# Three of the six hole-filling transfers of a later group move from ScalarE's program to SyncE's

## The reference

```python
for t in range(S):                                   # B, H, S, D = 4, 8, 768, 48
    cur = einsum('bhd,bhe->bhde', u[None] * kt, vt)
    y[:, :, t] = einsum('bhd,bhde->bhe', rt, state + cur)
    state = wt[..., None] * state + einsum('bhd,bhe->bhde', kt, vt)
x = y.transpose(0, 2, 1, 3).reshape(B * S, H * D)    # 3072 x 384
h = x @ w_in                                         # 384 x 2048
x = maximum(0.01 * h, h) @ w_out                     # 2048 x 384
# then: softmax over 8 experts by cosine / tau, argmax, and
out[mask] = gate_w[mask, None] * (maximum(x[mask] @ w1[e], 0) @ w2[e])   # F = 1024
```

## Time and profile before

| what | value |
|---|---|
| median of 3 runs | 859.35 us (857.68 to 860.33) |
| the profiled execution | 861.14 us |
| its span | 859.3 us, 17826 instructions |
| mean granted clock of PE | 0.993 |
| busy PE / DVE / ACT / POOL | 824.3 / 547.6 / 438.5 / 198.8 us |
| PE, L967 (1152 matmuls) and L988 (1152) | the first network, up to 573 us |
| PE, L1040 and L1076 | the experts, from 573 us to the end |

### The profile page before, as it was taken

One profiled execution on the slowest core, in us unless ns is written; L12 is line 12 of the kernel. 1 busy time (PEld: TensorE's weight loads), 2 busy tenths in 40 slices (PEclk: granted clock), 3 DMA queues, 4 the chain that ended last, 5 costly groups with the idle time before them and its releaser, 6 DMA issues.

```text
span 859.3 us, 17826 instructions
## 1 busy us (share of the span) xinstructions
PE 824.3 (96%) x5689; PEld 773.5 (90%) x5689; DVE 547.6 (64%) x1296; ACT 438.5 (51%) x919; POOL 198.8 (23%) x285
## 2 busy tenths in 40 slices
PE   5789999999999999999999999999999999999995
PEld 5689999999999999999999989999889988988885
DVE  6687598678778778878868855645461422454462
ACT  4565464364465455446446436554563534465472
POOL 5421011003012112112112001212323332423443
PEclk9999999999999999999999999999999999999998
DMA  8795221238122122112220000513531513285381
GB/s 176 160 233 127 52 65 39 44 76 89 38 69 38 39 60 56 39 24 69 44 43 30 2 15 29 167 37 102 193 112 40 186 38 131 98 295 181 110 275 49
DMA packets 141576, 78.81 MB, mean 92 GB/s; under 512 B 111566, under 2 KB 129525, under 8 KB 141362
## 3 DMA queue, kind: packets, MB, share of 16 engines
q1 hardware_dynamic: 134786, 64.69, 29.7%
q0 software_dynamic: 4544, 10.85, 3.8%
q10 hardware_dynamic: 2160, 2.21, 1.4%
HBM read 112.90 MB, written 11.63 MB: 145 GB/s over the span
## 4 chain that ended last, share of the span: by engine, by line
PE 79%; DVE 5%; DMA 3%; ACTq 3%; issue 3%; ACT 1%; SPq 0%; POOLq 0%; POOL 0%; DVEq 0%
PE bank L988 20%; PE bank L967 19%; PE bank L1076 12%; PE bank L1040 12%; ACTq L423 3%; PE bank L896 3%; PE bank L924 3%; PE bank L864 2%; PE bank L1057 2%; DMA xg<-x_moe,gi 2%; PE bank L919 2%; PE bank L904 1%; PE bank L1022 1%; DVE Xi L1527 1%; DVE Fi L1516 1%
## 5 line engine op out<-in xcount | busy, mean ns | idle before, releaser
L967 PE MATMUL bank<-xhl,WRh 128*128 128x384 f32 x768 | 218.7, 339 | 2.7 <-DMA xhl<-xhl 2.7
L967 PEld LDWEIGHTS bank<-xhl,WRh 128*128 128x128 f32 x768 | 141.4, 188 | 3.5 <-issue 2.0
L1311 ACT COPY gw<-bank 128x384 f32<-128x384 f32 x128 | 61.5, 481 | 155.1 <-PE bank L967 154.4
L988 PE MATMUL bank<-WRh,gh 128*128 128x384 f32 x384 | 136.4, 355 | 0.0
L967 PE MATMUL bank<-xhl,WRl 128*128 128x384 f32 x384 | 130.1, 339 | 0.0
L988 PE MATMUL bank<-WRh,gl 128*128 128x384 f32 x384 | 129.7, 338 | 0.0
L988 PE MATMUL bank<-WRl,gh 128*128 128x384 f32 x384 | 129.6, 338 | 0.0
L1597 DVE TENSOR_TENSOR gl<-gw,gh 128x384 fp32r<-128x384 f32 x128 | 76.2, 595 | 55.4 <-ACT gh L1317 51.9
L1590 DVE SCALAR_TENSOR_TENSOR gw<-gw 128x384 f32<-128x384 f32 x128 | 71.2, 556 | 61.5 <-ACT gw L1311 61.5
L1317 ACT CAST gh<-gw 128x384 fp32r<-128x384 f32 x128 | 65.4, 511 | 85.3 <-DVE gw L1590 59.4
L1765 DVE TENSOR_TENSOR hl<-bank,hh 128x512 fp32r<-128x512 f32 x56 | 36.1, 686 | 85.3 <-ACT hh L1352 83.4
(11 more groups left out here) (191 smaller groups left out, 1597.3 us busy)
## 6 DMA issues: line engine op xcount, KB each, us to landing
stage<-in_moe_w_dram SPq DMA_DIRECT2D x96, 768.0 KB
Wn<-in_w_dram SPq DMA_DIRECT2D x24, 192.0 KB, 2.6
Rn<-in_r_dram SPq DMA_DIRECT2D x24, 192.0 KB, 3.4
Kn<-in_k_dram SPq DMA_DIRECT2D x24, 192.0 KB, 3.5
Vn<-in_v_dram SPq DMA_DIRECT2D x24, 192.0 KB, 2.6
x_moe<-x2s SPq DMA_DIRECT2D x24, 192.0 KB, 2.8
wraw<-in_moe_w_out_dram SPq DMA_DIRECT2D x4, 768.0 KB, 7.8
eraw<-in_moe_w_dram SPq DMA_DIRECT2D x4, 768.0 KB, 9.7
```

Of the source, the lines that this page charges most:

```text
L967: mm = pe.matmul(bank[F_BANK[n % 2]][:, 0:GN], win(t_)[:, f // 4, k_, cols], xhl[G % 2][:, a, k_, :], start=(k_ == 0 and n_ == 0), stop=(k ...
L988: mm = pe.matmul(bank[O_BANK[i]][:, 0:DM], a[:, z, cols], wout(t_)[:, f, :], start=(f == 0 and n_ == 0), stop=(f == FT - 1 and n_ == 2))
L1311: act.copy(gw[:, n % 2, :], bank[F_BANK[n % 2]][:, 0:GN]).then_inc(s_g0, 1)
```

## The change

`fill` of SP is new: it waits for `s_yhi` and `s_ylo` of group g and issues `fill_half(sp, g, 1)`. It is called for group 0 where the same lines stood, and for groups 1 to 7 at the point of SP's program at which the third chunk's sums are due, ahead of `next_v`. ACT's `fill` loses its second `fill_half`. The number of transfers, their sizes and what waits for them (`s_fill`) are as before.

```diff
+            def fill(g):
+
+                sp.wait_ge(s_yhi, GT * (g + 1))
+                sp.wait_ge(s_ylo, GT * (g + 1))
+                fill_half(sp, g, 1)
...
-            sp.wait_ge(s_yhi, GT)
-            sp.wait_ge(s_ylo, GT)
-            fill_half(sp, 0, 1)
+            fill(0)
...
             for n in range(SECOND):
                 for m in at(sum_at, n - 1):
+                    if m % GT == GT - 1:
+                        fill(m // GT)
                     if m + NSLOT < NC:
                         next_v(m + NSLOT)
...
                 fill_half(act, g, 0)
-                if g > 0:
-                    fill_half(act, g, 1)
```

## The result

| | before | after |
|---|---|---|
| median, 6 runs each | 858.64 us (857.68 to 860.33) | 853.78 us (852.95 to 855.45) |
| ratio | | 0.9942, 95% interval 0.993 to 0.9953 |
| profiled execution, its span | 861.14, 859.3 us | 855.45, 853.7 us |
| PE from the matmul at 60.11 (61.89 after) to the first of the experts, below "the first stage" | 513.04 us | 508.20 us |
| from there to the end of the span | 286.2 us | 283.6 us |

A forecast was written before the change was run, and what follows sets the result against it. PE, with work for 96% of the span, was taken as the bound, its gaps hanging on ACT's six issues in a row. The gains 2.94 + 0.15 + 1.55 = 4.64 us, from 859.35, gave 854.7 us, range 852.6 to 857.8.

The forecast's parts named there:

- (a): Six gaps before PE's scores, behind the fills of groups 1 to 6: all closed, 2.94 us gained.
- (b): Start of group 6: the last fill lands 1.9 us earlier, 0.15 us gained.
- (c): Start of group 7: PE reads the flag and branches under running matmuls, 1.55 us gained.
- (d): SP issues three more fills in seven places, its load of v goes out 3.2 us later: cost 0.
- (e): Landing of fills issued by SP and ACT at once: still in time for PE, cost 0, bounds 0 and 0.9.
- Another holder of `Kt`: Before the scores: the six gaps stay, only 1.70 us gained, 857.7 us; chance 0.10.
- Nothing to be seen: Experts' stage: PE comes 4.6 us earlier but loses it to transfers keeping their own time, 859.35 us; chance 0.09.
- Flag not covered: Start of group 7: PE's sequencer can't branch ahead of its matmuls, gain there 0.56, 855.7 us; chance 0.16.
- Slower: Groups 1 to 6: ACT's fills and the load of v slow each other; 863.6 us with landings of 6; chance 0.05.

The follow-up runs named there:

- the held kernel: The changed kernel plus eight small copies on ACT behind its three fills, holding ACT for 1.76 us with no transfer; ratio 0.9961 to before.
- the one with the scans first: The kernel before, with DVE doing the decay scans ahead of the low part that waits for ACT, all six fills left on ACT; ratio 0.9972.

## Why the prediction was right

The time, 853.78 us, lies 0.9 us under the forecast of 854.7 and in the range. The forecast was taken from a median of before of 859.35, which six runs put at 858.64; against its own reference the gain was 4.86 us where 4.64 were forecast.

**(a) The gaps before the scores** were all closed, 2.28 + 0.64 = 2.92 us for 2.94. The reading of the chain from ACT's issue over DVE's low part to `Kt` was right, as the held kernel and the one with the scans first show from two sides. What I gave as the limit in groups 3 to 6, the router's products on DVE, was there, but tighter than I had it. Group 5 after, and below it `Kt` of the same group before:

```profile
371.65 1.90 ACTq L423 DMA_DIRECT2D xhl<-xhl  x3
374.81 0.08 DVE L1616 DVE_READ_ACCUMULATOR2_ANT logits<- 128x1 f32 x1
374.81 1.35 DVE L1603 TENSOR_TENSOR gl<-gw,gh 128x384 fp32r<-128x384 f32 x1
381.40 0.68 DVE L1550 TENSOR_TENSOR Kt<-bank,Xi 128x512 f32<-128x512 f32 x1
```

```profile
371.72 3.83 ACTq L423 DMA_DIRECT2D xhl<-xhl  x6
381.98 0.68 DVE L1544 TENSOR_TENSOR Kt<-bank,Xi 128x512 f32<-128x512 f32 x1
```

The low part starts 1.3 us earlier, as I had said, but directly behind the products it takes 1.35 us and not 0.56. From ACT's first issue, `Kt` comes 9.75 us later where it was 10.26, so only 0.51 us of ACT's 1.92 arrive, and not 1.25. It is the same in groups 3 and 4; in group 6, whose last issue had been stretched, it is 0.93. The gap was 0.46. PE's scores now start 0.20 us behind the end of `Kt` where they had waited until 0.15 behind it: in groups 3 to 6 there is 0.05 us to spare, and not the 0.79 that 1.25 would leave. In group 1, without the products, it is 1.46. That the gaps of groups 3 to 6 closed in full is in part luck. It is also why one transfer moved does as much there as three: in that kernel `Kt` of groups 3 to 6 comes at 9.73 or 9.74 us.

**(b) Group 6's start** gave its 0.15. The gap was put down to the landing, rightly, but not explained: it was an issue of 1.02 us, met by chance of the code's layout. Part of the 0.64 in (a) has the same source. These 0.3 us belong to the change as it is, and would not be there in a kernel whose code lies otherwise.

**(c) The branch** gave 1.56 us for 1.55. This was the step with two outcomes, and the one that I took came in: PE's sequencer read the flag and branched under nine matmuls. Choosing the flag and not the transfer that the profile names was right, and mattered: with the flag out of the way and the transfers as they were, PE waits 0.77 us less, which is how far apart the two paths ended.

**(d), (e) SP and the landings** cost nothing. SP's load of v was issued 3.4 us later (103.36 less the 1.78 of the whole picture, against 98.20), with no wait behind it. The cost of running beside the fills, which I bounded at 0 to 0.9, is 0.5 us of landing time and none of PE's. In that bound I took the issue of 1.02 us for what two sequencers cost each other. That was wrong: ACT issued alone there, and the packet above came with it. In group 0, where SP and ACT issue together, the longest was 0.81 us before and 0.87 after.

**The rivals.** "Another holder of `Kt`" is out by the gaps. "Nothing to be seen" is out by the time: the experts' stage did not get longer (286.2 us, then 283.6), and the kernel is faster, clear of the interval. "Flag not covered" is out: 0.17 us and not 1.2. "Slower" needed landings of 5.3 us; 3.3 was the longest. The rule that the prediction quotes from the Trainium skill ("DMA: Bandwidth & Descriptors", section "Issuing engines are not separate DMA queues"), that starting transfers from several engines saves only the sequencer's time, was weighed and set aside; the trace agrees with the rule itself, as the transfers got no faster (2.2 us, and 2.7 beside a load). It is its closing remark, that this time is small, that did not carry over: the whole gain came from 1.9 us of a sequencer's time, seven times.

## What to carry to other kernels

Issuing a transfer costs the engine that issues it as much as a small instruction, here 0.64 us each, and six in a row stand in that engine's program ahead of all that follows. Count such rows of issues as work where the engine has a deadline, and follow what its next instruction feeds, through the other engines' program order, until PE. What is won is the gap at the end of that path and no more, so one transfer of six gave most of it; what stands next on the path, here DVE's products, must be measured with the instruction behind it and not only up to its end; and where a wait names a transfer that landed 0.9 us earlier, look for the branch or the register load behind it.

## What the runs showed of the hardware

- A transfer that ACT issued within 0.24 us of the start of a packet of the instruction queue (queue 8) took 1.02 to 1.68 us to issue instead of 0.61, in each of the five kernels in which the two met; one of SP took 0.91 to 1.17 instead of 0.60 in three. When 81 instructions were put into TensorE's code, it hit another group.
- The DVE instruction directly behind a product and its accumulator read takes 1.35 us in groups 3 to 6 of the changed kernel, where the same one takes 0.56 after an idle of over 1 us.
- PE's sequencer can wait for a flag, read it (0.48 us) and branch under running matmuls with no loss, here with the flag written 1.55 us ahead of the first matmul behind the branch. Where the flag is late, PE starts 1.16 to 1.18 us after it, in six kernels.
- Fills of 48 KB from SBUF to SBUF land 0.5 us later beside a load of 192 KB from HBM on the other queue, and that load 0.7 us later beside them (2.6 to 3.3 us).
